# Token numbers carried as a column of the sorted rows, a last block ended tile by tile, and a block closed without GpSimd's drain

## The chip, the cores and the metric

The kernel runs on one core of one Trainium2 chip. The metric is the device time of one execution in microseconds (us). Matmuls run on TensorE (PE in the rows, its weight loads PEld), elementwise work on VectorE (DVE) and ScalarE (ACT); GpSimd (POOL) makes constants, splits weights and issues indirect DMAs; SyncE (SP) issues the plain DMAs. "q" behind an engine's name is its queue, that is its sequencer.

## The reference

Three stages in a row: a linear recurrence in the place of attention, a mixture of experts with one expert per token and a skip rule, and a dense two-layer part with SiLU.

```python
x = attn_out.transpose(0, 2, 1, 3).reshape(3072, 384)      # tokens
# experts
do_compute = x @ w_skip > 0
e_idx = argmax(x[do_compute] @ w_gate)                      # 8 experts
gate_w = softmax(...)[e_idx]
h = relu(x_e @ w1[e])                                       # 384 -> 1024
out = x; out[do_compute] += gate_w * (h @ w2[e])            # 1024 -> 384
# feed-forward
h = out @ w_in                                              # 384 -> 2048
y = (h / (1 + exp(-h))) @ w_out                             # 2048 -> 384
```

## The kernel before, in words

**Tokens and regions.** The 3,072 tokens lie as 24 tiles of 128 rows in `X`, each row 384 numbers and `EXTRA` = 8 more (the eight gate logits less their maximum). While attention still runs, `Routing` gives each token a row in `xs`, a DRAM buffer of nine regions: region 0 for tokens without an expert ("idle"), regions 1 to 8 for the experts. `scatter` (L176 to L181) sends each tile's rows there by one indirect DMA issued by GpSimd, in batches of six tiles and, at the end, 3, 2 and 1. `tabulate` (L187) writes a table from which the engines read, as register values, where each region's tokens go in the sorted order (`COLS_AT`) and how many passes of 224 rows are needed (one here).

**Experts** (`experts`, L1149). SP loads the first two experts' rows (`xt`), then the idle rows (`idle`, eight tiles of 224), and then, in `body` (L1259), weights and rows ahead: unit 2e is w1 of expert e, unit 2e+1 its w2, and three slots of `ring` hold them. `unit_ahead(P, u)` waits for the matmuls that read the slot's old unit and loads unit u. TensorE does for each expert `up` (48 matmuls, L1350), the turning of the next expert's rows, and `down` (48 matmuls in three columns of 16, L1364). VectorE (`keep`, L1459) multiplies each column by the gate and adds x into `kept`, which holds all tokens in sorted order. With the last expert's columns it also makes the feed-forward part's first inputs (`x_parts`, L1542). Meanwhile GpSimd splits w_in and w_out into 20 pieces of a high and a low part.

**Token numbers.** The output must leave in the original order, so the kernel needs for each sorted position the token's number. `find` (L222, VectorE, in expert 0) works out each token's sorted position. When the pieces are done and expert 6 is through (L1310), GpSimd issues 24 indirect DMAs (L1312), each writing 128 numbers of 4 bytes to `ids_dram`, waits until all have landed, and loads the 3,072 numbers into `ids` (L1316).

**Feed-forward** (`feed_forward`, L1509). Six blocks of four tiles (512 tokens). A block has 16 steps `up(b, f)` (nine matmuls of 512 columns, L1602) and 16 steps `down(b, f)` (three matmuls of 384 columns for each of the four tiles, L1612), with down two steps behind up. ScalarE reads each up result twice (g0, then the rounded gT, L1585 and L1590), VectorE makes the rest of gT (L1566). Up may run two steps ahead of ScalarE (two buffers pU), ScalarE four steps ahead of down (four buffers gT). A block ends with down 13, 14 and 15 in that order; the tiles are complete one after the other in down 15. VectorE copies each tile to `o` (L1574), and GpSimd stores it by an indirect DMA with the 128 numbers of `ids` (L1556). `gpsimd` of this part starts with a wait for `ids`.

**End.** All engines run in one `nc.Block()` (L1695). At its end GpSimd waits for its stores and drains; rows of this end carry the line 1645.

## Time and profile before

| | us |
|---|---|
| median of 3 runs | 918.07 |
| runs | 915.7, 918.07, 926.13 |
| profiled execution, its own time | 917.95 |
| its span, first to last instruction | 916.2 |
| TensorE busy | 841.4 (92%) |
| weight loads (PEld) busy | 773.2 |
| VectorE busy | 349.9 |
| ScalarE busy | 336.5 |
| GpSimd busy | 173.4 |

Attention takes up the first 300 us, the experts run to 484 us, the feed-forward part to 904 us. A busy share is an average over these stages: what a change is worth is read from the stage in which it lies and from what is waited for there last. A row in order of time tells when a group of equal instructions started, for how long it ran (a matmul's end is modelled), and in brackets how long the engine had idled before and what released it. "remote" there means that the profile found no instruction or queue of this core that the release could be put down to.

### The profile page before, as it was taken

The numbers are of one execution on the slowest core, as the hardware profiler recorded it, in microseconds if no ns is written. First come the engines' busy times: TensorE is split into PE (matmuls) and PEld (weight loads), VectorE is DVE, ScalarE is ACT, GpSimd is POOL, SyncE is SP. The second block draws the span as 40 slices with busy tenths as digits, with TensorE's granted clock in tenths as the row PEclk, the third lists the DMA queues.
The fourth block names the chain that finished last, engine by engine and source line by source line (L and its number), as shares of the span: only waits on it lengthen the run. The fifth ranks groups of instructions, "written<-read, shape, count | busy, mean of one in ns | idle before, by whom it ended". The sixth has DMA issues, their size and how long they took to land.

```text
span 916.2 us, 12820 instructions
## 1 busy us (share of the span) xinstructions
PE 841.4 (92%) x5092; PEld 773.2 (84%) x5092; DVE 349.9 (38%) x669; ACT 336.5 (37%) x564; POOL 173.4 (19%) x218
## 2 busy tenths in 40 slices
PE   1499999999999499999995899999999999999994
PEld 0388998899899389999994789899999989898984
DVE  1688768768664331222221122222132122132111
ACT  6888778778532120011110222222222222222220
POOL 2210111412303233433457001001001001001001
PEclk9799999999999789999999899999999999999998
DMA  9999568655522385676520000000000000000000
GB/s 173 168 221 213 77 87 126 125 65 87 143 95 96 117 221 191 204 237 230 184 93 0 1 1 16 20 1 26 9 1 35 1 1 35 1 1 35 1 0 35
DMA packets 168182, 77.28 MB, mean 84 GB/s; under 512 B 145608, under 2 KB 161320, under 8 KB 168112
## 3 DMA queue, kind: packets, MB, share of 16 engines
q1 hardware_dynamic: 162352, 60.48, 31.2%
q0 software_dynamic: 5760, 15.86, 5.2%
q8 instruction: 45, 0.74, 0.3%
q14 instruction: 25, 0.20, 0.1%
HBM read 60.77 MB, written 15.56 MB: 83 GB/s over the span
## 4 chain that ended last, share of the span: by engine, by line
PE 88%; ACT 3%; DVE 3%; issue 2%; DMA 2%; another core or an unknown queue 2%; POOL 1%; DVEq 0%; SPq 0%; POOLq 0%; ACTq 0%
PE f_pU L1602 22%; PE f_pO L1612 22%; PE e_pH L1350 8%; PE e_pY L1364 7%; PE sc L515 5%; PE yp L546 4%; PE yp L545 4%; PE kvp L529 3%; PE tq L499 2%; PE tk L504 2%; PE cs L474 2%; PE cs L112 2%; PE cs L487 1%; PE cs L488 1%
## 5 line engine op out<-in xcount | busy, mean ns | idle before, releaser
L1602 PE MATMUL f_pU<-f_xT,wi 128*128 128x512 f32 x864 | 218.9, 400 | 13.8 <-ACT gT L1590 8.2
L1612 PE MATMUL f_pO<-wo,gT 128*128 128x384 f32 x1152 | 214.4, 336 | 0.0
L1612 PEld LDWEIGHTS f_pO<-wo,gT 128*128 128x128 f32 x1152 | 203.2, 188 | 7.7
L1602 PEld LDWEIGHTS f_pU<-f_xT,wi 128*128 128x128 f32 x864 | 163.5, 191 | 46.8 <-ACT gT L1590 8.5
L1566 DVE TENSOR_TENSOR gT<-g,gT 128x512 fp32r<-128x512 f32 x96 | 66.5, 692 | 302.6 <-ACT gT L1590 289.4
L1585 ACT ACTIVATE g<-f_pU 128x512 f32<-128x512 f32 x96 | 57.5, 599 | 317.7 <-PE f_pU L1602 305.2
L1556 POOL DMA_INDIRECT out<-o,ids_in x24 | 24.1, 1002 | 372.2 <-DVE o L1574 366.8
L1350 PE MATMUL e_pH<-e_xT,ring 128*128 128x224 f32 x384 | 75.8, 358 | 0.0
L1350 PEld LDWEIGHTS e_pH<-e_xT,ring 128*128 128x128 f32 x384 | 74.1, 194 | 0.3
L1364 PE MATMUL e_pY<-hT,ring 128*128 128x224 f32 x384 | 74.1, 353 | 0.0
L1364 PEld LDWEIGHTS e_pY<-hT,ring 128*128 128x128 f32 x384 | 72.1, 190 | 0.0
L546 PE MATMUL yp<-vraw,SK 128*128 128x48 f32 x384 | 70.0, 274 | 0.2 <-issue 0.2
L1411 ACT ACTIVATE hT<-e_pH 128x448 f32<-128x448 f32 x32 | 17.4, 544 | 131.9 <-PE e_pH L1350 131.9
L545 PE MATMUL yp<-U,QT 96*128 96x48 f32 x320 | 59.3, 267 | 0.4 <-ACT store L699 0.4
L546 PEld LDWEIGHTS yp<-vraw,SK 128*128 128x128 f32 x384 | 56.9, 191 | 2.2 <-issue 0.3
L1590 ACT ACTIVATE gT<-f_pU 128x512 fp32r<-128x512 f32 x96 | 56.9, 593 | 0.0
L515 PE MATMUL sc<-QT,KT 96*128 96x128 f32 x384 | 52.7, 280 | 0.3 <-ACT QT L692 0.3
L515 PEld LDWEIGHTS sc<-QT,KT 96*128 96x128 f32 x384 | 48.3, 193 | 4.7 <-ACT QT L692 1.1
L545 PEld LDWEIGHTS yp<-U,QT 96*128 96x128 f32 x320 | 49.0, 191 | 2.2 <-ACT store L699 0.6
L474 PE MATMUL cs<-LM,tri 128*128 128x384 f32 x48 | 22.6, 561 | 21.3 <-DVE LM L783 17.4
L499 PE MATMUL tq<-ident,QN 128*96 128x128 f32 x192 | 29.3, 275 | 10.0 <-DVE KN L814 10.0
L180 POOL DMA_INDIRECT xs<-store,slots x24 | 28.2, 1177 | 52.2 <-DVE slots L174 33.3
(185 smaller groups left out, 963.8 us busy)
## 6 DMA issues: line engine op xcount, KB each, us to landing
ring<-in_moe_w SPq DMA_DIRECT2D x16, 1536.0 KB, 7.8
ring<-in_a_re SPq DMA_DIRECT2D x8, 576.0 KB, 7.6
ring<-in_a_im SPq DMA_DIRECT2D x8, 576.0 KB, 8.4
ring<-in_q SPq DMA_DIRECT2D x8, 576.0 KB, 8.2
ring<-in_k SPq DMA_DIRECT2D x8, 576.0 KB, 8.3
vraw<-in_v SPq DMA_DIRECT2D x8, 576.0 KB, 4.7
xs<-zero SPq DMA_DIRECT2D x9, 343.0 KB, 7.2
part<-in_moe_w_in POOLq DMA_DIRECT2D x12, 256.0 KB, 5.2
```

What stands on the lines that cost most here:

```text
L474: pe.matmul(cs[j % 2][:, 0:PW], tri[:, :], piece(LM, j), start=True, stop=True).then_inc(s["sum_l"], 1)
L499: mm = pe.transpose(tq[0:D2, h, :], QN[g % 2][:, h * NC + c, :], ident[:, :])
L515: mm = pe.matmul(sp_[n % 2][:, h, :], KT[n % 2][0:D2, h, :], QT[n % 3][0:D2, h, :], start=True, stop=True)
L545: pe.matmul(y, QT[n % 3][0:D2, h, :], U[c % 2][0:D2, h, :], start=True, stop=False)
L546: mm = pe.matmul(y, SK[n % 2][:, h, :], vraw[g % 2][:, h * NC + c, :], start=(c == 0), stop=True)
L1350: mm = pe.matmul(pH[i % 2][:, f % 2 * TILE:(f % 2 + 1) * TILE], w1[:, c * FF + f * 128:c * FF + (f + 1) * 128], xT[:, e % 2, c, :], start= ...
L1364: mm = pe.matmul(pY[:, c, 0:TILE], w2[:, f * DM + c * 128:f * DM + (c + 1) * 128], hT[:, f, :], start=(f == 0), stop=(f == NF - 1))
L1566: dve.tensor_tensor(g[:, 1, :], g0[:, f % 2, :], g[:, 0, :], ALU.subtract).then_inc(s["g_out"], 1)
L1585: act.activation(g0[:, f % 2, :], pU[f % 2][:, :], ACT.Silu)
L1590: act.activation(gT[f % GB][:, 0, :], pU[f % 2][:, :], ACT.Silu).then_inc(s["g_hi"], 1)
L1602: mm = pe.matmul(pU[f % 2][:, :], wi[:, pw, c, f * 128:(f + 1) * 128], xT[b % 2][:, px, c, :], start=(k == 1), stop=(k == NK * len(TERMS)))
L1612: mm = pe.matmul(pO[t][:, 0:DM], gT[f % GB][:, pg, t * 128:(t + 1) * 128], wo[:, pw, f, :], start=(f == 0 and k == 0), stop=(f == NF - 1 a ...
```

## The change

Each row in `X` and `xs` gets a ninth extra number, the token's own number as a float, written once by an iota. It is scattered with the row. Sorted token numbers then come out of `xs` itself: `move_ids`, on SP's queue, copies the last column of the idle rows (1,792 numbers) and of each expert's first 224 rows (eight copies) to their place in `ids_dram`, each after the one before has landed, since a copy's tail is overwritten by the next. Then SP loads the 3,072 numbers to `ids`; VectorE converts them to integers (`row_of`) in block 0. `find`, the 24 indirect writes and GpSimd's load are gone. In the last block, up 14 and up 15 come without a down between them, then down 12, and then downs 13 to 15 tile by tile. The block is closed with `no_gpsimd_drain=True`. The branch for more than one pass, which doesn't run here, gets its own moves.

```diff
-EXTRA = 8
+EXTRA = 9
...
-        pool.iota(self.ids, pattern=[[128, self.NT]], base=0, channel_multiplier=1)
+        pool.iota(self.X[:, :, self.DM + self.E:self.DM + self.E + 1], pattern=[[128, self.NT], [0, 1]], base=0,
+                  channel_multiplier=1, allow_small_or_imprecise_dtypes=True)
...
-    def find(self, dve, s, wide, moved):
-
-        ALU, AX = mybir.AluOpType, mybir.AxisListType
-        shift = bass.AP(self.shift.tensor, self.shift.offset, [self.shift.ap[0], [0, self.NT], self.shift.ap[1]])
-        dve.scalar_tensor_tensor(self.shift, self.base, 128.0, self.start, ALU.mult, ALU.subtract)\
-            .then_inc(s["find_step"], 1)
-        dve.wait_ge(s["find_step"], 1)
-        dve.tensor_tensor(wide, self.hot, shift, ALU.mult).then_inc(s["find_step"], 1)
-        dve.wait_ge(s["find_step"], 2)
-        dve.tensor_reduce(moved, wide, AX.X, ALU.add).then_inc(s["find_step"], 1)
-        dve.wait_ge(s["find_step"], 3)
-        dve.tensor_tensor(self.found, self.row, moved, ALU.subtract).then_inc(s["find_step"], 1)
...
+            def move_ids(r, P, e):
+
+                j = e + 1 if e < E else 0
+                if isinstance(r, int):
+                    row = slice(j * REGION, j * REGION + TILE)
+                    at = bass.ds(column(sp, slice(COLS_AT + j, COLS_AT + j + 1)), TILE)
+                    if e == 0:
+                        sp.wait_ge(more["ids_moved"], 16)
+                    else:
+                        sp.wait_ge(P["ids_moved"], 16 * e)
+                else:
+                    row = bass.ds(sp.value_load(table[0:1, bass.ds(r * routing.R + (ROWS_AT + j), 1)],
+                                                min_val=0, max_val=routing.R * REGION - TILE), TILE)
+                    at = bass.ds(column(sp, bass.ds(r * routing.R + (COLS_AT + j), 1)), TILE)
+                    sp.wait_ge(P["ids_moved"], r * (16 * routing.R) + 16 * (1 + e - routing.R))
+                sp.dma_start(ids_dram[at, :], xs[row, ROW - 1:ROW], allow_slow_non_contiguous=True)\
+                    .then_inc(P["ids_moved"], 16)
...
                     unit_ahead(P, 2 * e + 4)
+                    move_ids(r, P, e)
...
+            sp.dma_start(ids_dram[0:FIRST_IDLE * TILE, :], xs[0:FIRST_IDLE * TILE, ROW - 1:ROW],
+                         allow_slow_non_contiguous=True).then_inc(more["ids_moved"], 16)
...
+            sp.wait_ge(last["ids_moved"], 16 * E)
+            sp.dma_start(ids.rearrange("p (n o) -> p n o", o=1),
+                         ids_dram[0:routing.PAD, :].rearrange("(n p) o -> p n o", p=128),
+                         allow_slow_non_contiguous=True).then_inc(s["ids_in"], 16)
...
-            pool.wait_ge(s["find_step"], 4)
-            pool.wait_ge(last["down_done"], NK * (E - 1))
-            for n in range(routing.NT):
-                pool.indirect_dma_start(ids_dram, bass.IndirectOffsetOnAxis(ap=routing.found[:, n:n + 1], axis=0),
-                                        routing.ids[:, n:n + 1], None, bounds_check=routing.PAD - 1, oob_is_err=False)\
-                    .then_inc(s["ids_out"], 16)
-            pool.wait_ge(s["ids_out"], 16 * routing.NT)
-            pool.dma_start(ids.rearrange("p (n o) -> p n o", o=1), ids_dram.rearrange("(n p) o -> p n o", p=128),
-                           allow_slow_non_contiguous=True).then_inc(s["ids_in"], 16)
...
-                    wide = tmp[:, :, :].rearrange("p a t -> p (a t)")
-                    NW = routing.NT * routing.R
-                    routing.find(dve, s, wide[:, 0:NW].rearrange("p (n e) -> p n e", e=routing.R),
-                                 wide[:, NW:NW + routing.NT])
...
-            pool.wait_ge(e_s["ids_in"], 16)
+            pool.wait_ge(s["row_done"], 1)
             for n in range(NT):
                 pool.wait_ge(s["o_out"], n + 1)
-                pool.indirect_dma_start(out, bass.IndirectOffsetOnAxis(ap=ids[:, n:n + 1], axis=0), o[:, n % TB, :], None,
+                pool.indirect_dma_start(out, bass.IndirectOffsetOnAxis(ap=row_of[:, n:n + 1], axis=0), o[:, n % TB, :], None,
...
+                if b == 0:
+                    dve.wait_ge(e_s["ids_in"], 16)
+                    dve.tensor_copy(row_of[:, :], ids).then_inc(s["row_done"], 1)
...
-            def down(b, f):
+            def down(b, f, t):
+                for k, (pg, pw) in enumerate(TERMS):
+                    mm = pe.matmul(pO[t][:, 0:DM], gT[f % GB][:, pg, t * 128:(t + 1) * 128], wo[:, pw, f, :],
+                                   start=(f == 0 and k == 0), stop=(f == NF - 1 and k == 2))
+                if f == NF - 1:
+                    mm.then_inc(s["tile_done"], 1)
+                return mm
+
+            def down_all(b, f):
                 pe.wait_ge(s["g_out"], b * NF + f + 1)
                 for t in range(TB):
                     if f == 0 and b > 0:
                         pe.wait_ge(s["o_out"], (b - 1) * TB + t + 1)
-                    for k, (pg, pw) in enumerate(TERMS):
-                        mm = pe.matmul(pO[t][:, 0:DM], gT[f % GB][:, pg, t * 128:(t + 1) * 128], wo[:, pw, f, :],
-                                       start=(f == 0 and k == 0), stop=(f == NF - 1 and k == 2))
-                    if f == NF - 1:
-                        mm.then_inc(s["tile_done"], 1)
+                    mm = down(b, f, t)
                 if f < NF - 1:
                     mm.then_inc(s["down_done"], 1)
+
+            def down_last(b, first):
+
+                for t in range(TB):
+                    for f in range(first, NF):
+                        if t == 0:
+                            pe.wait_ge(s["g_out"], b * NF + f + 1)
+                        down(b, f, t)
...
                     up(b, f)
-                    if f >= 2:
-                        down(b, f - 2)
-                down(b, NF - 2)
-                down(b, NF - 1)
+                    if f >= 2 and (b < NB - 1 or f < NF - 2):
+                        down_all(b, f - 2)
+                if b < NB - 1:
+                    down_all(b, NF - 2)
+                    down_all(b, NF - 1)
+                else:
+                    down_all(b, NF - 4)
+                    down_last(b, NF - 3)
...
-    ids_dram = nc.dram_tensor("sorted_ids", (NT * 128, 1), I32, kind="Internal").ap()
+    ids_dram = nc.dram_tensor("sorted_ids", (NT * 128 + TILE, 1), F32, kind="Internal").ap()
...
-        ids = sb("ids_in", [128, NT], I32)
+        ids = sb("ids_in", [128, NT])
...
-        block = ctx.enter_context(nc.Block())
+        block = ctx.enter_context(nc.Block(no_gpsimd_drain=True))
```

## Rows read from the trace of the kernel before

**Rows 1.** The page's first line: the span and the number of instructions.

```profile
span 916.2 us, 12820 instructions
```

**Rows 2.** Table by stage: stretch, length, busy us (instructions) per engine, PEclk, DMA share, GB/s.

```profile
480.00:510.00 30.00, 16.16 (x65) 13.18 (x64) 6.11 (x12) 3.15 (x6) 18.11 (x19) 0.82 0.02 0
...
570.00:900.00 330.00, 330.00 (x1657) 297.84 (x1656) 76.21 (x120) 86.98 (x160) 19.50 (x20) 1.00 0.03 13
```

**Rows 3.** Order of time, TensorE: start, us, engine, line, tiles, shapes, count, [idle before].

```profile
474.57 9.24 PE L1364 MATMUL e_pY<-hT,ring 128*128 128x224 f32 x48
...
483.49 1.73 PE L1602 MATMUL f_pU<-f_xT,wi 128*128 128x512 f32 x6
...
489.32 4.53 PE L1602 MATMUL f_pU<-f_xT,wi 128*128 128x512 f32 x12 [4.11 <-DVE f_xT L1550]
...
508.04 4.21 PE L1602 MATMUL f_pU<-f_xT,wi 128*128 128x512 f32 x9 [8.15 <-ACT gT L1590]
...
568.95 6.45 PE L1602 MATMUL f_pU<-f_xT,wi 128*128 128x512 f32 x27
...
635.87 4.36 PE L1602 MATMUL f_pU<-f_xT,wi 128*128 128x512 f32 x18
```

**Rows 4.** Order of time, VectorE and ScalarE at the hand-over.

```profile
487.15 0.39 DVE L1462 TENSOR_TENSOR e_tmp<-e_pY,gB 128x224 f32<-128x224 f32 x1 [4.21 <-remote]
...
488.57 0.69 DVE L1550 TENSOR_TENSOR f_xT<-store,f_xT 128x512 fp32r<-128x512 f32 x1
...
494.30 0.60 ACT L1585 ACTIVATE g<-f_pU 128x512 f32<-128x512 f32 x1 [17.68 <-PE f_pU L1602]
...
506.90 0.60 ACT L1585 ACTIVATE g<-f_pU 128x512 f32<-128x512 f32 x1 [11.52 <-remote]
```

**Rows 5.** Order of time, GpSimd: first and last of 24 indirect writes, then the load.

```profile
472.95 1.08 POOL L1312 DMA_INDIRECT sorted_ids<-ids,found  x1 [0.16 <-issue]
...
502.62 0.98 POOL L1312 DMA_INDIRECT sorted_ids<-ids,found  x1 [0.30 <-issue]
510.62 1.48 POOL L1316 DMA_DIRECT2D ids_in<-sorted_ids  x1 [7.02 <-DMA sorted_ids<-ids,found]
```

**Rows 6.** Order of time, the end: four copies to o, first and last of four stores.

```profile
902.19 2.12 DVE L1574 COPY o<-f_pO 128x384 f32<-128x384 f32 x4 [2.89 <-PE f_pO L1612]
903.55 0.98 POOL L1556 DMA_INDIRECT out<-o,ids_in  x1 [61.96 <-DVE o L1574]
...
907.40 0.98 POOL L1556 DMA_INDIRECT out<-o,ids_in  x1 [0.30 <-issue]
```

**Rows 7.** Line 1645 by instruction: form, count, min/median/max ns, first and last start us.

```profile
L1645 POOLq COMPARE_BRANCH  x1: 43/43/43, 910.1 to 910.1; - x1
L1645 POOLq DRAIN  x1: 5712/5712/5712, 910.2 to 910.2; - x1
```

**Rows 8.** Order of time, ScalarE in attention, behind six row scatters.

```profile
294.09 0.59 ACT L692 ACTIVATE QT<-tq 96x512 f32<-96x512 f32 x1 [4.80 <-remote]
```

**Rows 9.** Order of time, VectorE's first instruction after find.

```profile
333.47 0.39 DVE L1472 COPY store<-e_pX 128x224 f32 x1 [4.62 <-PE e_pX L1375]
```

**Rows 10.** DMA issues: tiles, queue, kind, count, KB each, median us from issue to landing.

```profile
ring<-in_moe_w SPq DMA_DIRECT2D x16, 1536.0 KB, 7.8
...
xt<-xs SPq DMA_DIRECT2D x8, 343.0 KB, 8.1
...
fend_all<-chunk_ends SPq DMA_DIRECT2D x16, 4.5 KB, 2.7
...
ids_in<-sorted_ids POOLq DMA_DIRECT2D x1, 12.0 KB, 5.1
```

**Rows 11.** Order of time, TensorE: the first layer of experts 6 and 7.

```profile
446.29 9.24 PE L1350 MATMUL e_pH<-e_xT,ring 128*128 128x224 f32 x48
...
465.49 9.24 PE L1350 MATMUL e_pH<-e_xT,ring 128*128 128x224 f32 x48
```

**Rows 12.** DMA queues from 472 to 512 us: packets, MB, share of 16 engines.

```profile
q8 instruction: 1, 0.02, 0.1%
```

More of the change, by code:

```diff
@@ L37, in __init__ @@
         self.slots = sb("slots", [128, NT], I32)
-        self.found = sb("found", [128, NT], I32)
-        self.ids = sb("ids", [128, NT], I32)
         self.row = sb("row", [128, NT])
@@ L47, in __init__ @@
         self.start = sb("start", [128, R])
-        self.shift = sb("shift", [128, R])
         self.table = sb("table", [1, 288], I32)
@@ L1132, in __init__ @@
         self.s = {n: sem(prefix + n) for n in """xt_in0 xt_in1 turned ex_done gate_step diag_done gB_done gB_out xT_out
-            up_done h_out down_done y_read wb_step kept idle_act w0 w1 w2""".split()}
+            up_done h_out down_done y_read wb_step kept idle_act ids_moved w0 w1 w2""".split()}
         self.r = r
@@ L1195, in experts @@
         s = {n: sem("e_" + n) for n in """idle_in0 idle_in1 idle_turned idle_dve again part_in part_hi part_lo
-            find_step ids_out ids_in""".split()}
+            ids_in""".split()}
         table = routing.table
@@ L1282, in sync @@
                     sp.wait_ge(w_here[u], 16)
+                sp.wait_ge(more["ids_moved"], 16)
                 routing.tails(sp, after["table_done"], s["again"], xs)
@@ L1287, in sync @@
                         body(r, P)
+                        move_ids(r, P, IDLE)
+                        sp.wait_ge(P["ids_moved"], r * (16 * routing.R) + 16)
                         sp.wait_ge(P["idle_act"], r)
@@ L1532, in feed_forward @@
         g0 = sb("g0", [128, 2, N])
+        row_of = sb("row_of", [128, NT], mybir.dt.int32)
         o = sb("o", [128, TB, DM])
@@ L1537, in feed_forward @@
         pO.append(pb(f"f_pO{TB - 1}", [128, N]))
-        s = {n: sem("f_" + n) for n in """x_hi x_out up_done g_hi g_out down_done tile_done o_out stored0 stored1 stored2
+        s = {n: sem("f_" + n) for n in """x_hi x_out up_done g_hi g_out down_done tile_done o_out row_done stored0 stored1 stored2
             stored3""".split()}
```

## Prediction, made before the changed kernel was run

> **What bounds the kernel now.** I read the page first: span 916.2 us [rows 1]. The profiled execution took 917.95 us, so 1.75 us lie around the span; the median of the three runs is 918.07, near enough that the sum below, made against 917.95, needs no shift. The table by stage comes next. From 570 to 900 us TensorE is busy 330.00 of 330.00 us at a granted clock of 1.00 (2.4 GHz), so there only fewer matmuls would help, and the change takes none away. In 480 to 510 us, where the experts hand over to the feed-forward part, it is busy 16.16 of 30 us [rows 2]. That is the hole in the kernel.
>
> Its size, from the order of time: the first matmuls of the feed-forward blocks 0, 1 and 2 start at 483.49, 568.95 and 635.87 us [rows 3]. Block 1 took 66.92 us (blocks 2 to 4 step alike), block 0 took 85.46 us with the same matmuls. Block 0 loses 18.54 us.
>
> Who is late? VectorE takes expert 7's last column at 487.15, after 4.21 us waiting for something the profile calls "remote", though the matmuls that release it ended at 483.81. ScalarE starts on the first unit at 494.30, though its nine matmuls (six before 485.21, three from 489.32) were issued by about 490.5, and on the second at 506.90, 11.52 us "remote", though TensorE had ended it at 493.85 and had gone on [rows 3, 4]. TensorE then sat until 508.04 for ScalarE's result; its granted clock fell meanwhile (0.82 over the window). So nobody lacked work or an operand: semaphores of TensorE that had been due were seen late.
>
> What else ran? GpSimd issued the 24 indirect writes of token numbers (L1312) from 472.95 to 503.60, one per 1.28 us. It goes on at 510.6, 7.0 us after the last issue, when all have landed [rows 5]; the output's last store is seen landed 2.7 us after it starts (907.40 to 910.1) [rows 6, 7]. Signals are late on this queue too, and ScalarE runs again 3.3 us after GpSimd's last issue. The same sign stands at one more place only: at 294.09 ScalarE ends a wait of 4.80 us for "remote" [rows 8], just behind a burst of six row scatters (L180). My reading: a long burst of indirect DMAs holds back the semaphores of the other engines.
>
> **The change, part by part.**
>
> *find removed (VectorE, L226 to L233).* Four small instructions. Behind them VectorE idles 4.62 us for TensorE until 333.47 [rows 9]. Worth 0; were that idle time gone, at most four times 0.4 us, by the larger copy of that row.
>
> *24 indirect writes removed.* The issue time is GpSimd's own, and it has nothing else to do before the first output store. What counts is block 0. If no signal is late, VectorE starts the last column at 483.83 and needs 2.12 us (487.15 to 488.57 plus 0.70 [rows 4]), so TensorE, out of work at 485.21 (489.32 less 4.11), goes on at 485.96. That 0.75 us wait stays. Behind it each wait is covered: ScalarE's two passes take 1.1 us (506.90 to 508.04) while TensorE spends 66.92/32 = 2.1 on the next unit. Gain 18.54 - 0.75 = **17.8 us**. Bounds: 0 (the burst is not the cause) and 18.5. I take 17.8, since the late signals of this stretch, on two engines and a DMA queue, all lie in or just behind the burst, and the only other ones at another burst.
>
> *The moves on SP.* One copy of 1,792 single elements in DRAM behind the eight idle loads; eight of 224, each behind a weight load and a wait for the previous move; one of 3,072 into SBUF, which GpSimd did before. None appears in the trace. Nearest rows: 1,152 single elements land in 2.7 us, 3,072 in 5.1 [rows 10]. So at most 2.7 for a short one and some 3.5 for the long one. On SP's queue behind the long one stand the x load of expert 2 (wanted two experts later) and weight unit 3; behind a short one, weight unit 2e+5. A unit is asked for when the matmuls that read its slot end, and wanted 19.2 us later, one expert period (446.29 to 465.49 [rows 11]); it lands in 7.8 us [rows 10], so 11.4 us of slack hide all this. The end of this chain: up of expert 6 ends at 455.5, unit 15 lands by 463.7, two moves and the load back follow by about 474, wanted in block 0's tail near 551. SP also computes register values and waits; it has nothing else to do. Cost 0; without the cover, 2.7 per expert.
>
> The Trainium skill (DMA: Bandwidth & Descriptors, section Rules for kernel authors) speaks against this part: a last dimension that isn't contiguous becomes one descriptor per element. The trace agrees as far as a 12 KB transfer needs 5.1 us where 1,536 KB need 7.8; by the rule the moves are dear per byte, and the sum stays as it is, since there are few bytes.
>
> *Rows of 393 numbers for 392.* Scatter, loads and blanks move 0.26% more. The one load on the path, the first xt, lands in 8.1 us [rows 10]; 0.26% of that is 0.02 us. Rows now start at multiples of 4 bytes, not 32; no row shows a price, bounds 0 to 0.8 us (a tenth of that landing), I take 0. iota into X: one small instruction for another.
>
> *row_of and its wait on VectorE.* A copy of 128x24, under the 0.39 us of one of 128x224 [rows 9], in front of the block 0 copies, for which VectorE idles on TensorE anyhow. Queued behind: those copies, then GpSimd. Cost 0, as the ids are 75 us early.
>
> *The last block by tiles.* Matmul count and TensorE's end stay. Now tile 0 is done at 902.17 (its copy starts 902.19) and the others 0.52 us apart, so TensorE ends at 903.74. GpSimd needs 1.28 us per store (0.98 and 0.30), starts 0.79 us after the first copy's end (902.76 to 903.55), and the fourth store begins at 907.40, which is TensorE's end E + 3.66 [rows 6]. With tiles 1.57 us apart (nine matmuls of 0.174) the queue never builds: last copy ends E + 0.59, store begins E + 1.38. Gain 3.66 - 1.38 = **2.3 us**. The moved up(14), up(15) meet buffers freed by down 10 and 11: ScalarE's 1.1 and VectorE's 0.69 us are covered by 2.1 us of down(12) and more of tile 0. Bounds 1.5 to 2.8 (a copy or wait more or less, 0.79 against 0.30).
>
> *No drain.* After the last store's landing (branch at 910.1) GpSimd's DRAIN starts at 910.2 and takes 5.71 us, and the span ends at 916.2 behind it [rows 1, 7]. All bytes have landed, no other engine works. Gain **5.7 us**; bounds 0 (something else takes the time up) and 5.7. I take 5.7, as nothing else runs that could end last.
> Here the Trainium skill (VectorE: DVE Perf Modes, section The DRAIN you can't avoid) says that the DRAINs of preamble and postamble take a constant 12 ns or so on all engines. By that this part would be worth nothing. The row shows 5,712 ns, and it decides.
>
> Sum: 917.95 - 17.8 - 2.3 - 5.7 = **892.2 us**.
>
> **Rivals.**
> - *The hand-over stall is not the burst's.* Another cause, such as instruction loading or the first use of new code, would keep it. Against: from 472 to 512 us the instruction queue shows one packet [rows 12], and it passed in the first microsecond; the stall ends with the burst. For: the two bursts of six row scatters before that one show no "remote" wait, nor do the output's bursts of four. Time: 917.95 - 2.3 - 5.7 = 910.0.
> - *A rest of it stays,* as large as the small burst's late signal, 4.8 us [rows 8]: 897.0. For: no row shows what carries the signals, and SP now sends small packets in this stretch. Against: the 3,072-element load that followed the burst at 510.6 brought none.
> - *The drain's 5.7 us come back* in what ends the program (outside the span, say): 897.9. The 1.75 us now outside would grow.
> - *Slower than before: moves hold the weights.* Each short move stands ahead of a weight unit on one queue and SP waits for the one before. The unit issues 9.2 us after the move (48 matmuls [rows 11]), the load ahead takes 7.8, the slack is 11.4: from 9.2 - 7.8 + 11.4 = 12.8 us per move on, each further microsecond costs one per expert, six times. To eat the 25.8 us, a move must take 12.8 + 4.3 = 17 us; at 20 us the time is 892.2 + 6 x 7.2 = 935. Against: 1,152 elements in 2.7 us; but those ran from DRAM to SBUF or back, never DRAM to DRAM.
>
> **Numbers.** Forecast 0.72, whole stall stays 0.09, rest of it 0.08, drain comes back 0.08, slower 0.03. The forecast's own range is 890.5 to 894.5 (the 0.75 us wait, 1.5 to 2.8 at the tail, 0 to 0.8 for alignment). The range goes on to the two rivals near 898 with the scatter of runs (915.7 for 918.07 below, as much above): 889 to 899.5; left out are the stall that stays, the slower case and tails. About 1% is what a measurement can tell: faster means below 908.9. Faster 0.72 + 0.08 + 0.08 = 0.88; same 0.09 (910.0 is 0.9% below); slower 0.03.
>
> **What would show it.** Right: blocks 0 and 1 start 67.7 us apart and ScalarE's unit waits hold no "remote" near the hand-over; GpSimd has no work between its last weight piece and the first output store; the last store starts some 1.4 us after TensorE's end; no DRAIN of 5.7 us, and some 4.5 us from TensorE's end to the span's. Wrong: block 0 still some 85 us with ScalarE late; TensorE waiting for `ring` loads between experts; 1.75 us outside the span grown to 7; a store queue at the end.

## The result, and the profile after

The changed kernel takes 910.5 us in the median of 20 runs (906.04 to 920.54), the kernel before 920.32 us beside it (914.91 to 926.32). The ratio is 0.9891, with a 95% interval of 0.9864 to 0.9919. That is 9.8 us between the medians, where the prediction had 25.8 (917.95 less 892.2), and 910.5 lies outside its range of 889.0 to 899.5. The executions of one kernel scatter by about 1%, in the kernel before mostly around 918 to 920 or near 926.

The profiled execution took 911.48 us. TensorE in order of time, from the last expert to the second block of the feed-forward part (start, us, what, and in brackets the idle time before it):

```profile
span 909.7 us, 12820 instructions
```

```profile
471.02 9.24 PE L1355 MATMUL e_pH<-e_xT,ring 128*128 128x224 f32 x48
480.10 9.24 PE L1369 MATMUL e_pY<-hT,ring 128*128 128x224 f32 x48
500.90 8.86 PE L1607 MATMUL f_pU<-f_xT,wi 128*128 128x512 f32 x27 [11.56 <-POOL wo L1322]
570.23 6.45 PE L1607 MATMUL f_pU<-f_xT,wi 128*128 128x512 f32 x27
```

The hole at the hand-over [rows 3] has changed its owner. No late semaphore is left there. Instead TensorE stands idle for 11.56 us in front of block 0, and what releases it is GpSimd, splitting its last piece of `wo`. The last expert also starts 5.53 us later than before (471.02 for 465.49). The span that the prediction implies is 890.45 us (892.2 less 1.75), so 19.25 us too many are to be found. Expert 7 has 5.53 of them. From expert 7 to block 0 it is 29.88 us where before it was 18.00, which makes 11.88. Block 0 lasts 69.33 us for the 67.67 that were predicted: its first 27 matmuls take 8.86 us where block 1's take 6.45, 2.41 more at a granted clock of 0.77 in the stretch of 480 to 510 us, and the 0.75 us of waiting that the prediction had inside the block is not there. That is 1.66. The end of the kernel has the other 0.2.

Why is GpSimd late? It loads the feed-forward weights in 20 pieces into one buffer (`part`), and for each it waits until the load has landed. Its waits (total us, times, longest), and TensorE's for it:

```profile
POOL wi L1320 <- DMA part<-in_moe_w_in: 80.1, 12, 10.2
POOL wo L1320 <- DMA part<-in_moe_w_out: 41.2, 8, 8.4
PE f_pU L1607 <- POOL wo L1322: 11.6, 1, 11.6
```

The same waits in the kernel before:

```profile
POOL wi L1306 <- DMA part<-in_moe_w_in: 55.3, 12, 7.2
POOL wo L1306 <- DMA part<-in_moe_w_out: 39.7, 8, 7.0
```

That is 26.3 us more over 20 loads, and the last piece's CAST (the first of the two instructions that split it) starts at 498.2 instead of 470.1, 28.1 us later. This lateness alone sets the start of block 0. In the kernel before, the last piece was done at 472.8 and block 0 started at 483.49, so 10.7 us of the 28.1 are hidden and 17.4 are not (500.90 for 483.49). The experts' 5.53 us lie under the same wait and are not a second loss.

The DMA issues of the changed kernel (KB each, median us to landing), to be laid beside [rows 10]:

```profile
ring<-in_moe_w SPq DMA_DIRECT2D x16, 1536.0 KB, 10.0
part<-in_moe_w_in POOLq DMA_DIRECT2D x12, 256.0 KB, 7.5
...
sorted_ids<-xs SPq DMA_DIRECT2D x8, 0.9 KB, 10.6
sorted_ids<-xs SPq DMA_DIRECT2D x1, 7.0 KB, 16.2
ids_in<-sorted_ids SPq DMA_DIRECT2D x1, 12.0 KB, 5.2
```

The pieces of w_in in the kernel before:

```profile
part<-in_moe_w_in POOLq DMA_DIRECT2D x12, 256.0 KB, 5.2
```

A short move takes 10.6 us where I had said at most 2.7, the long one 16.2 where I had said 3.5, and the large loads beside them take longer as well: 7.5 us for 5.2 a piece of w_in, 10.0 for 7.8 a unit of the ring. The clearest row is that of the DMA queues (packets, MB, share of 16 engines' time) from 408 to 485 us; q0 is GpSimd's, with the pieces. First the changed kernel:

```profile
q1 hardware_dynamic: 9761, 11.33, 50.3%
q0 software_dynamic: 832, 2.88, 29.4%
```

and the kernel before:

```profile
q1 hardware_dynamic: 4560, 9.79, 37.8%
q0 software_dynamic: 1056, 2.76, 10.6%
```

q0 moves nearly the same bytes (before, the first indirect writes are among its packets), but its packets are in the engines for 2.8 times as long. All packets of that stretch, the changed kernel's and then the kernel before's:

```profile
DMA packets 10599, 14.29 MB, mean 186 GB/s; under 512 B 4457, under 2 KB 8833, under 8 KB 10593
```

```profile
DMA packets 5621, 12.61 MB, mean 164 GB/s; under 512 B 495, under 2 KB 3904, under 8 KB 5616
```

Not all of the 4,457 small packets count against the moves: some 3,000 are those of the load of 3,072 numbers to `ids`, which starts only at 480.8. Up to 480.7 us the changed kernel has 1,456 packets under 512 bytes and the kernel before 385, and the shares of q0 are 27.9% and 11.1% already. So it is about a thousand small packets, those of five short moves, that go with the longer loads.

The end came out as predicted. The last copy and the last store, and GpSimd's last row:

```profile
905.11 0.56 DVE L1579 COPY o<-f_pO 128x384 f32<-128x384 f32 x1 [1.03 <-PE f_pO L1613]
```

```profile
906.46 0.98 POOL L1558 DMA_INDIRECT out<-o,row_of  x1 [0.61 <-issue]
```

```profile
L1666 POOLq COMPARE_BRANCH  x1: 43/43/43, 909.1 to 909.1; - x1
```

The last store starts 1.38 us after TensorE's end (905.08), and the span ends 4.6 us after TensorE's end, where it was 12.5 before.

### The profile page after: what moved, and what is told of

It reads as the page before. It is cut to its first block, busy times and chain, and to the rows that moved or that the text cites. A ratio compares the mean times of both kernels' runs of the same rounds, so it can differ in the third digit from the quotient of the medians.

```text
span 909.7 us, 12820 instructions
## 1 busy us (share of the span) xinstructions
PE 843.3 (93%) x5092; PEld 776.3 (85%) x5092; DVE 354.7 (39%) x666; ACT 336.4 (37%) x564; POOL 150.1 (16%) x193
## 4 chain that ended last, share of the span: by engine, by line
PE 71%; DMA 16%; POOL 6%; issue 3%; ACT 2%; DVE 2%; SPq 0%; POOLq 0%; DVEq 0%; ACTq 0%
PE f_pU L1607 22%; PE f_pO L1613 22%; DMA part<-in_moe_w_in 9%; DMA part<-in_moe_w_out 5%; PE sc L501 5%; PE yp L532 4%; PE yp L531 4%; PE kvp L515 3%; PE tq L485 2%; PE tk L490 2%; PE cs L460 2%; POOL wi L1322 2%; PE cs L110 2%; POOL wo L1322 2%; PE cs L473 1%
## 5 line engine op out<-in xcount | busy, mean ns | idle before, releaser
L1558 POOL DMA_INDIRECT out<-o,row_of x24 | 24.2, 1008 | 382.4 <-DVE o L1579 376.0
L1369 PE MATMUL e_pY<-hT,ring 128*128 128x224 f32 x384 | 76.2, 360 | 0.0
L1369 PEld LDWEIGHTS e_pY<-hT,ring 128*128 128x128 f32 x384 | 74.0, 195 | 0.4
L1416 ACT ACTIVATE hT<-e_pH 128x448 f32<-128x448 f32 x32 | 17.4, 543 | 133.6 <-PE e_pH L1355 133.6
L460 PE MATMUL cs<-LM,tri 128*128 128x384 f32 x48 | 22.7, 561 | 21.2 <-DVE LM L769 17.3
```

The costliest lines, as they stand in the source:

```text
L460: pe.matmul(cs[j % 2][:, 0:PW], tri[:, :], piece(LM, j), start=True, stop=True).then_inc(s["sum_l"], 1)
L1369: mm = pe.matmul(pY[:, c, 0:TILE], w2[:, f * DM + c * 128:f * DM + (c + 1) * 128], hT[:, f, :], start=(f == 0), stop=(f == NF - 1))
```

## The experiments

The runs fell on four numbered chips, and the chip turned out to matter: on chips 0 and 1 the kernel before takes 919.9 and 920.3 us, on chips 7 and 10 ("quick" below) it takes 900.5 and 901.1. Each ratio is that of a version to the kernel before on the same chip; where two versions are compared across chips, this is said or the chips are named. The chip of the first comparison isn't recorded; by its 920.3 it is of the first kind.

**All nine moves behind the last piece (chips 7 and 1), called "nine late" below.**

```diff
                     unit_ahead(P, 2 * e + 4)
-                    move_ids(r, P, e)
...
-            sp.dma_start(ids_dram[0:FIRST_IDLE * TILE, :], xs[0:FIRST_IDLE * TILE, ROW - 1:ROW],
-                         allow_slow_non_contiguous=True).then_inc(more["ids_moved"], 16)
...
             body(0, last)
+            sp.wait_ge(s["part_lo"], len(pieces))
+            sp.dma_start(ids_dram[0:FIRST_IDLE * TILE, :], xs[0:FIRST_IDLE * TILE, ROW - 1:ROW],
+                         allow_slow_non_contiguous=True).then_inc(more["ids_moved"], 16)
...
+            for e in range(E):
+                move_ids(0, last, e)
```

> The changed kernel, but all nine moves of token numbers are issued only when GpSimd has split its 20th weight piece. Theory M (the moves, 6,656 single elements through the DMA engines, slow the weight pieces that GpSimd waits for one by one): the last piece is done near 473 us as before, TensorE starts block 0 near 483 to 486 us, block 0 takes some 67.7 us with no late semaphore, and the time is 892 us against 918 (ratio 0.972). Rival W (the rows of 393 numbers are what slows the loads): the last piece stays near 500 us and the time near 911 (0.989). Rival H (the stall of before belongs to the hand-over, not to the burst of indirect DMAs): pieces on time, but ScalarE late again in 483 to 508 us: about 910.

On chip 7: 892.81 us beside 900.49, ratio 0.9916 [0.9898, 0.9933]. The time is the expected one, the ratio (0.972) isn't, because the kernel before is faster on this chip. The last piece is split at 470.3 again, and TensorE waits 0.81 us for VectorE at the hand-over and for nobody else.

> The first experiment again, with all nine moves behind the last piece. Theory (two separate things: what the moves cost, and a stall of the kernel before that some chips have): where the kernel before takes about 901 us the ratio is again 0.9916; where it takes about 918 us, with the late semaphores in its trace, this kernel has no such stall and the ratio is about 0.972 to 0.975, 893 to 895 us. Rival (the slower chip is slower for other reasons, and its stall comes back elsewhere without the burst): the ratio there is 0.98 or more.

On chip 1: 895.57 us beside 920.26, ratio 0.9727 [0.9678, 0.9776], as the theory had it. TensorE there:

```profile
484.14 1.73 PE L1611 MATMUL f_pU<-f_xT,wi 128*128 128x512 f32 x6
486.68 5.16 PE L1611 MATMUL f_pU<-f_xT,wi 128*128 128x512 f32 x21 [0.81 <-DVE f_xT L1556]
```

Nine transfers behind one another on SP and the load back, 71 us in all (473.1 to 544.1 on chip 7), cost nothing there: nobody needs the ids before the first store. This version beats both kernels on either kind of chip (for the changed kernel across chips: 892.81 on chip 7, 907.64 on chip 10), and it is the one to keep.

**Only the eight short moves late (chip 7).** The long move stays in its early place.

```diff
-                    move_ids(r, P, e)
...
             body(0, last)
+            sp.wait_ge(s["part_lo"], len(pieces))
...
+            for e in range(E):
+                move_ids(0, last, e)
```

> As the kernel with all moves late, but the long move (1,792 numbers, idle rows) stays where the change put it, behind the idle loads. Theory M in the form that the number of elements counts: half of the 3,584 moved elements are early, so about half of the lateness of the last piece stays, done near 486 us: block 0 starts near 486 and the time is 893 to 897. In the form that each short move hurts by standing ahead of or beside a weight load: the last piece near 476 us, 892. Rival W: near 500 us, 911.

896.99 us, ratio 0.9946 [0.9930, 0.9963]; 4.2 us over all nine late. The long move lands in 16.1 us beside the idle loads, TensorE waits 1.77 us for one of them, and expert 7 starts at 470.59 instead of 465.50. There is no wait for a piece: the last one is cast at 475.5. So the expected time (893 to 897) was met, but not by the expected way, a last piece that is late (486).

**The changed kernel itself on a quick chip (chip 10).** No edit.

> The changed kernel itself, unaltered, beside the kernel before on one chip. Where the kernel before took 900.5 us, its hand-over had no late semaphore, so the change has no 17.8 us to win there. Theory (the late semaphores of the kernel before belong to some chips only, and the moves cost what they cost everywhere): moves late gave 892.8 us there; with the moves where the change puts them the last piece of weights is late as in the profiled run of the changed kernel (498 us against 470), TensorE waits some 8 to 11 us for it at the hand-over and the experts end 5 us later, so 892.8 + 10 to 16 = 903 to 909 us, a ratio of 1.003 to 1.01: the change loses or ties where the stall is absent. Rival A (the moves cost only what the eight short ones and the long one showed one by one: 4.2 us for the long one): about 897 to 900, ratio below 1. Rival B (the stall is in every run of the kernel before, and its time differs between chips for another reason): the ratio is again 0.989.

907.64 us beside 901.13, ratio 1.0078 [1.0055, 1.0101]. On this chip the change makes the kernel slower. TensorE's wait for the last piece is 12.12 us. The idle tiles come in time here although the long move takes 15.0 us, and expert 7 starts at 467.05; the loss is the late piece alone (cast at 494.8).

**The kernel before itself, for its trace (chip 10).** No edit.

> The kernel before itself, for its trace on this chip. Theory (the stall belongs to the chip): where it takes about 900 us, the hand-over rows of VectorE and ScalarE show no wait of 4.2 and 11.5 us put down to a late semaphore, and blocks 0 and 1 of the feed-forward take the same 67 us; where it takes about 918 us they show them, and block 0 takes 85 us. Rival (the 18 us between the chips are lost elsewhere): the waits of 4.2 and 11.5 us are there at 900 us too, and the missing time is in another stretch.

902.35 us, and its waits hold no "remote" at all. The 24 writes start from 482.19 to 512.81, straight across the hand-over, and TensorE passes it undisturbed:

```profile
486.73 1.72 PE L1602 MATMUL f_pU<-f_xT,wi 128*128 128x512 f32 x6
489.53 5.16 PE L1602 MATMUL f_pU<-f_xT,wi 128*128 128x512 f32 x21 [1.08 <-DVE f_xT L1550]
```

So the late semaphores of [rows 4], and the small one of [rows 8] too, belong to one kind of chip.

**Each short move made twice (chip 10).**

```diff
                 sp.dma_start(ids_dram[at, :], xs[row, ROW - 1:ROW], allow_slow_non_contiguous=True)\
                     .then_inc(P["ids_moved"], 16)
+                if isinstance(r, int):
+                    sp.wait_ge(P["ids_moved"], 16 * (2 * e + 1))
+                    sp.dma_start(ids_dram[at, :], xs[row, ROW - 1:ROW], allow_slow_non_contiguous=True)\
+                        .then_inc(P["ids_moved"], 16)
```

> The changed kernel with each of the eight short moves made twice, one after the other, to the same place (the output stays the same). Theory (each short move holds back the pieces of weights that GpSimd waits for, about 28 us of lateness at the last piece over nine moves, 3 us a move): the last piece's cast comes another 20 to 25 us late, at about 520 us, TensorE waits another 20 us for it, and the time is 20 us or more over the changed kernel's own in this call. Rival (the moves share the bandwidth only, 0.9 KB each): the second set costs under 2 us. Rival (the price is the wait on SP, not the transfer): TensorE waits for the ring's weights within the experts instead, and the last piece keeps its time.

938.11 us, ratio 1.0395 [1.0366, 1.0423]: 30.5 us over the changed kernel on the same chip, where 20 or more were expected. The last piece is cast at 525.3 instead of 494.8, which is the same 30.5, and the waits are now of two kinds:

```profile
PE f_pU L1611 <- POOL wo L1326: 22.7, 1, 22.7
...
PE e_pY L1373 <- DMA ring<-in_moe_w: 12.1, 5, 4.8
```

The second is the one that the slower rival of the prediction named, and it needed two moves per expert. It makes expert 7 start 19.4 us later (486.50 for 467.05), but TensorE has to wait for the last piece after that all the same.

**Other transfers at the nine places (chip 1).** The real moves are late, and at the old places transfers of as many bytes go in unbroken runs (seven of 256 numbers for the long move, one of 224 for each short one).

```diff
+            def like_ids(rows, e, n):
+                at = routing.PAD + TILE + (e % 2) * TILE if rows == 1 else routing.PAD + 3 * TILE
+                sp.dma_start(ids_dram[at:at + rows * n, :].rearrange("(r n) o -> r (n o)", r=rows),
+                             xs[e * REGION:e * REGION + rows, 0:n]).then_inc(last["ids_moved"], 16)
...
                     unit_ahead(P, 2 * e + 4)
-                    move_ids(r, P, e)
+                    if isinstance(r, int):
+                        sp.wait_ge(last["ids_moved"], 16 * (e + 1))
+                        like_ids(1, e, TILE)
...
+            like_ids(7, 0, 256)
```

> All nine real moves go behind the last piece of weights, as in the first experiment, and at the nine old places in SP's queue stand transfers of the same bytes in unbroken runs of numbers (seven runs of 256 for the long one, one run of 224 for each short one) into a spare part of the scratch memory, with the same waits between them. Theory (the price comes from the single elements, one small packet each, 3,584 of them): these nine cost nearly nothing, the last piece is cast at about 471 us and the ratio is that of moves late, 0.9916, within 0.3%. Rival (any transfer from memory to memory at those nine places of the queue, or the wait before it, costs this): the last piece is cast near 498 us, ratio 1.005 to 1.01.

894.50 us, ratio 0.9704 [0.9655, 0.9753], no different from all nine late on the same chip. Queue q0 from 408 to 485 us:

```profile
q0 software_dynamic: 896, 3.15, 12.9%
```

With nine late it is 12.6% for the same 896 packets. (The profiled execution is one that enters the experts some 7 us later, so its times from the start of the span don't compare; the share does.) Neither the place in the queue, nor the waits before it, nor the bytes cost anything that these runs can tell. The single elements do.

**The eight short moves early, the long one not (chip 0).** All nine are made late too, so that the result stays whole, and the early eight go to a spare place.

```diff
+            def like_ids(e):
+                j = e + 1 if e < E else 0
+                at = routing.PAD + TILE + (e % 2) * TILE
+                sp.dma_start(ids_dram[at:at + TILE, :], xs[j * REGION:j * REGION + TILE, ROW - 1:ROW],
+                             allow_slow_non_contiguous=True).then_inc(last["ids_moved"], 16)
...
                     unit_ahead(P, 2 * e + 4)
-                    move_ids(r, P, e)
+                    if isinstance(r, int):
+                        sp.wait_ge(last["ids_moved"], 16 * e)
+                        like_ids(e)
```

> All nine real moves behind the last piece, and beside them the eight short ones made as well at their old places, into a spare part of the scratch memory; the long one has no early twin. Theory (prices add: the long move 4.2 us, the eight short ones the rest of the 14.8 us between the changed kernel and the one with moves late on the quick chips): about 10 us over moves late, 903 us, last piece cast near 490 us. Rival (it takes the long move to put the chain behind; the short ones alone fit in its slack of 12.6 us at the last piece): 893 to 896 us, last piece cast before 483 us.

907.67 us, ratio 0.9875 [0.9838, 0.9912], 12.1 over nine late on chip 1, where about 10 were expected. The last piece is cast at 493.0, 22.1 us later than there, 2.8 per move. 10.6 us of that are its slack at the hand-over; for the rest TensorE waits:

```profile
PE f_pU L1621 <- POOL wo L1336: 11.8, 1, 11.8
```

and the experts keep their times (expert 7 at 465.58). The load back of the 3,072 numbers is late here too, so it isn't needed for the effect. The short moves do this alone, 12.1 of the 14.9 us. What the long one adds depends on what is waited for last: with the short ones late it is the experts' delay (4.2 us), in the changed kernel, where that delay lies under the wait for the piece, it is a last piece cast still later (498.2 for 493.0; 2.8 us between the medians, 14.9 less 12.1).

**Two buffers for the pieces (chip 0).** The moves stay where the change has them.

```diff
-        part = sb("part", [128, 768])
+        part = sb("part", [128, 2, 768])
...
+                load_piece(i + 1)
+                pool.wait_ge(s[f"part_in{i % 2}"], 16 * (i // 2 + 1))
```

> The changed kernel, moves where it has them, with two buffers for the pieces of weights instead of one: GpSimd issues the load of the next piece before it splits the one at hand. Theory (the moves hurt because GpSimd's chain is load, wait, split, load, so that every longer load adds to it): the chain has room again, the last piece is cast before the hand-over, TensorE's wait for it there (12.1 us in the changed kernel) is gone, and what stays over the kernel with moves late is the experts' later end, 4 to 6 us. On a chip where the kernel before takes 901 us this gives 896 to 899 us, ratio 0.995 to 0.998; where it takes 920 us, 897 to 901, ratio about 0.976. Rival (the DMA engines themselves are full, so pieces that start earlier only take longer, and the ring's weights and x with them): the last piece or the experts are as late as before and the time is within 1% of the changed kernel's, 907 to 910 us.

901.57 us, ratio 0.9792 [0.9736, 0.9847], about 9 us under the changed kernel's 910.5. GpSimd's last split starts at 421.8 instead of 499.1, and its waits have shrunk:

```profile
POOL wi L1329 <- DMA part<-in_moe_w_in: 27.7, 8, 6.4
POOL wo L1329 <- DMA part<-in_moe_w_out: 17.0, 6, 4.9
...
PE e_pX L1389 <- DMA idle<-xs: 4.1, 1, 4.1
```

Each piece's load still takes 7.4 to 7.6 us. So the engines weren't short of time for the pieces; it was the chain of load, wait, split with one buffer that added up every delay. The collision at the idle tiles stays: from expert 0 to expert 1 it is 35.1 us where nine late has 28.1. Those 7 us are the 6 us between the medians by which this version is behind it (901.57 for 895.57 on chip 1).

**Rows of 393 numbers alone (chip 1).** The rest is as in the kernel before.

```diff
-EXTRA = 8
+EXTRA = 9
...
+        pool.iota(self.X[:, :, self.DM + self.E:self.DM + self.E + 1], pattern=[[128, self.NT], [0, 1]], base=0,
+                  channel_multiplier=1, allow_small_or_imprecise_dtypes=True)
```

> The kernel before with rows of 393 numbers, the ninth extra number being the token's own; found, burst and the rest stay. Theory (the length of the rows costs 0 to 0.8 us): ratio 1.000 within its interval, the last piece keeps its cast at about 470 us and the experts their times. Rival (rows of 1572 bytes instead of 1568 slow the scatter or the loads of x, and are part of why the changed kernel's experts end 5 us later): the writes of the rows or the loads of x are visibly longer, 3 to 6 us more in all.

919.11 us, ratio 1.000 [0.9971, 1.0030]. The last piece is cast at 470.2 and expert 7 starts at 465.37, as before. No price, as far as an interval of 2.7 us to either side can tell.

**The drain alone (chip 10).** One edit to the kernel before.

```diff
-        block = ctx.enter_context(nc.Block())
+        block = ctx.enter_context(nc.Block(no_gpsimd_drain=True))
```

> The kernel before with one edit: the block is closed without GpSimd's drain. Theory (the 5712 ns drain lay on the path behind the last store): the time falls by 5.7 us, ratio about 0.9937, and the engines' last rows show no drain on GpSimd. Rival (the drain only covered what takes place anyway, so another engine's closing work ends last): it falls by less than 2 us.

894.24 us, ratio 0.9931 [0.9907, 0.9955], 6.9 us between the medians. GpSimd's closing rows hold no DRAIN, and the span ends 0.4 us after its branch.

**The last block by tiles alone (chip 1).** One edit to the kernel before, as the change has it.

```diff
-                down(b, NF - 2)
-                down(b, NF - 1)
+                if b < NB - 1:
+                    down_all(b, NF - 2)
+                    down_all(b, NF - 1)
+                else:
+                    down_all(b, NF - 4)
+                    down_last(b, NF - 3)
```

> The kernel before with one edit: the last block ends tile by tile. Theory (the last store starts 1.38 us after TensorE's end instead of 3.66, GpSimd's drain stands behind it as before): 2.3 us less, ratio about 0.9975. Rival (the drain waits out what the earlier stores leave, so an earlier last store is lost in it): no change, ratio 1.000. If this chip is one where the kernel before takes about 918 us, its trace shows the late semaphores at the hand-over here too, since the burst is untouched.

916.18 us, ratio 0.9958 [0.9929, 0.9987]: 1.2 to 6.5 us faster, with the predicted 2.3 inside. The last store starts 1.39 us after TensorE's end. The stall is in this trace, with the burst untouched:

```profile
ACT g L1585 <- remote: 28.6, 2, 19.1
...
PE f_pU L1602 <- DVE f_xT L1550: 6.3, 1, 6.3
PE f_pU L1602 <- ACT gT L1590: 6.1, 1, 6.1
DVE e_tmp L1462 <- remote: 5.8, 1, 5.8
```

**The burst behind the sixth unit of block 0 (chips 7 and 0).** The 24 writes of the kernel before and their load stand in a function `numbers`, which GpSimd calls in the feed-forward part.

```diff
         def gpsimd(pool):
+            pool.wait_ge(s["up_done"], 6)
+            e_s["numbers"](pool)
             pool.wait_ge(e_s["ids_in"], 16)
```

> The kernel before, but the burst of 24 indirect writes is issued only when TensorE has done the sixth up of block 0 (near 505 us), unpaced. Theory B: the hand-over is clean (block 0's first six steps without 'remote'), and the late semaphores come inside the burst, some 505 to 540 us; block 0 still takes 80 to 86 us and the time stays near 918. Rival H: the stall stays at 483 to 508 us and none comes later.

On chip 7: 900.87 us, ratio 1.0004 [0.9991, 1.0018], no late semaphore. That chip has no stall to move, so it told nothing of its cause.

> The kernel before with its 24 indirect writes behind the sixth up step of block 0 instead of at the hand-over. Only of use on a chip where the kernel before takes about 920 us. Theory (while the 24 writes are queued, a semaphore that is not seen to arrive holds an engine that waits for another engine, wherever the writes stand): late semaphores stand inside block 0 now, 500 to 540 us, and the time stays at 915 to 920 us, ratio near 1.0. Rival (the stall needs writes and hand-over together, with its semaphores between all engines at once): no late semaphore, 902 us or below, ratio 0.98. Where the kernel before takes 901 us both say 1.000.

On chip 0: 918.14 us beside 919.89, ratio 0.9993 [0.9959, 1.0026]. The hand-over is clean, and the stall has gone with the burst (513.56 to 544.3). ScalarE, in order of time:

```profile
521.13 0.60 ACT L1591 ACTIVATE g<-f_pU 128x512 f32<-128x512 f32 x1 [3.10 <-issue]
...
530.76 0.60 ACT L1591 ACTIVATE g<-f_pU 128x512 f32<-128x512 f32 x1 [8.54 <-PE f_pU L1608]
...
547.75 0.60 ACT L1591 ACTIVATE g<-f_pU 128x512 f32<-128x512 f32 x1 [15.91 <-remote]
```

The units before and after come every 4.18 us, with 3.1 of idle time. Here 26.6 us pass for two. Block 0 lasts 84.62 us (492.49 to 577.11; this profiled execution enters the experts late, so its times are shifted) where nine late on chip 1 has 68.16. The stall has followed the writes to this place.

**A wait for the landing after each of the 24 writes (chip 7).** An edit to the kernel before.

```diff
                     .then_inc(s["ids_out"], 16)
+                if n % 1 == 0:
+                    pool.wait_ge(s["ids_out"], 16 * (n + 1))
```

> The kernel before, but GpSimd waits for each of the 24 indirect writes of token numbers to land before it issues the next. Theory B (a pile of indirect DMAs in flight holds back the other engines' semaphores): no wait for 'remote' at the hand-over, block 0 takes some 68 us in place of 85.5, the time is 918 - 17.8 = 900 (ratio 0.981). Rival H (the hand-over itself stalls): block 0 stays at 85 us, ratio 1.00. Rival B2 (each such DMA delays signals by some amount, whether or not others are in flight): stalls spread over 473 to 566 us, ratio near 1.00.

915.18 us, ratio 1.0149 [1.0124, 1.0174]. None of the three expectations came true: no wait is "remote", and the kernel is slower. A write that is waited for takes 5.3 us of waiting in the mean (122.1 over 23) beside the 0.98 of its issue, where without waiting they follow each other every 1.28; the ids come in at 624.7 only, and the output's copies then wait for their buffers, and TensorE once for 12.6 us behind them:

```profile
POOL sorted_ids L1312 <- DMA sorted_ids<-ids,found: 122.1, 23, 8.2
```

```profile
DVE o L1576 <- DMA out<-o,ids_in: 20.5, 4, 18.3
```

The run tells what spacing costs; what it would save couldn't show on this chip.

## Why the prediction missed

*Removing the 24 writes, 17.8 us.* Right for the kind of chip whose trace I had. Before minus nine late is 24.7 us on chip 1 and 7.7 on chip 7; the end of the kernel is in both, so the stall is worth 17.0. By the traces it is 17.3: block 0 lasts 85.46 us in the kernel before and 68.16 with nine late on chip 1. Its cause was the burst, as read from [rows 3 to 5]: shifted, it takes the stall along. That another chip has none could not be seen in one trace.

*Drain 5.7, tiles 2.3.* Right: together 7.7 us between the medians on chip 7 (before to nine late), each alone faster by an interval that holds its figure. The drain alone measured 6.9 us between medians, with 4.1 to 8.4 as its interval. The Trainium skill (VectorE: DVE Perf Modes, section The DRAIN you can't avoid) puts the DRAINs of preamble and postamble at some 12 ns on all engines. GpSimd's here belongs to the block, since it is gone when the block is closed without it; it took 5,712 ns [rows 7], so the page's figure doesn't hold for it.

*Rows of 393, find, row_of.* Rows of 393 measure 0, as taken. The other two show nothing in any trace.

*The moves on SP, "Cost 0".* This is the step that failed, by 14.8 us: 907.64 less 892.81 on the quick chips (10 and 7), 14.9 by 910.5 less 895.57 on the others. Without it the forecast holds: nine late has ratio 0.9727 [0.9678, 0.9776] on chip 1, and 892.2 is 0.9719 of 917.95. It failed twice. The first fault is the size. A short move was put at 2.7 us by a row of 1,152 single elements between DRAM and SBUF [rows 10], on a queue with nothing beside it. From DRAM to DRAM, in a stretch where weights stream, 224 elements take 10.6. The second fault is larger. I looked for cover only where the moves stand, on SP's queue, and found 11.4 us of slack for the ring's units. That was even right: TensorE never waits for them in the changed kernel, only with two moves per expert. But the transfers of one queue hold up those of another (q0's packets took 27.9% of the engines' time for 11.1%, with q1's single elements beside them), and another client had too little slack. GpSimd's 20 pieces go one at a time through one buffer, last 152 us (320.6 to 472.8), and end 10.7 us ahead of their use. Nine moves made them 28.1 us late, and two buffers in place of one took TensorE's wait for them away with the moves where they were. I did not ask who else was loading. A row of before held it (the pieces' waits, 55.3 and 39.7 us), and the prediction doesn't name it.

The prediction quoted the rule that speaks against this part (the Trainium skill, DMA: Bandwidth & Descriptors, section Rules for kernel authors: a last dimension that isn't contiguous becomes a descriptor per element) and kept the cost at nothing, "since there are few bytes". The runs agree with the rule: from 408 to 485 us nine late has 6,608 packets on q1 where the kernel before has 4,560, about one more for each of the 2,016 elements of the long and the first short move. As many bytes in unbroken runs cost nothing. Bytes were the wrong measure; packets were the right one.

*The forecast's own range.* Its terms give 891.0 to 893.8 us, not 890.5 to 894.5; nothing hung on that.

*The rivals.* The slower one named the right agent, the moves, with the wrong victim. Its point of decision, 12.8 us per expert for the moves ahead of a unit, holds as far as two runs can tell: one move of 10.6 brings no wait for the ring, two of 8.2 one behind the other (16.4) bring 12.1 us of it and start expert 7 19.4 us later, where its rule gives 6 x 3.6 = 21.6. The time was near that of "the stall isn't the burst's" (910.0), but that is luck: the stall was gone, and a wait that I had not priced took its place.

What stays open: what makes the two kinds of chip, and what carries the semaphores that are late on one of them. Four numbered chips split two and two; no row tells them apart but these. An early long move goes with a wait for the idle tiles in four traces (1.0 to 4.1 us) but not in that of the changed kernel on chip 10; why was not looked into. That it is the number of packets and not the step of 1,572 bytes between the elements was not tested apart.

## What to carry to other kernels

Before small transfers are put among large ones, count their packets, not their bytes, and look for the client of the DMA engines with the least slack, on whatever queue: above all one that loads, waits and computes through a single buffer. Put such transfers where nothing streams. And a stall read from one trace may be that chip's own, so take the trace of the kernel before on the chip on which the change is judged.

## What the hardware showed that I had not expected

- Single elements from DRAM to DRAM (medians of a run): 224 land in 6.5 to 6.9 us behind the last piece and in 10.6 to 11.0 among weight loads, 1,792 in 8.8 to 9.7 and in 15.0 to 18.5. One of the short ones costs a neighbour's chain of waited loads 2.8 us.
- On chips 0 and 1 a burst of 24 indirect writes costs the other engines some 17 us; on chips 7 and 10 the same instructions cost none. On chip 0 it is not only semaphores: inside the burst TensorE starts its matmuls one at a time, mostly with 0.7 to 1.6 us put down to "issue" ahead of each:

```profile
541.36 0.58 PE L1608 MATMUL f_pU<-f_xT,wi 128*128 128x512 f32 x1 [1.33 <-issue]
542.76 0.58 PE L1608 MATMUL f_pU<-f_xT,wi 128*128 128x512 f32 x1 [0.82 <-issue]
```

- An indirect write whose landing is waited for before the next costs about 6.3 us (0.98 and a wait of 5.3 in the mean); 24 in a row without waiting take 1.28 each.
